# Windowed attention scores on one Trainium2 core: a block-diagonal 128x128 product becomes two 64x64 products, one for each head

## What is computed

```python
# attention: q, k, v are (4, 8, 576, 64) float32, batch x heads x positions x width
scores = scale * np.matmul(q, k.transpose(0, 1, 3, 2))
rel = pos[:, None] - pos[None, :]
mask = (rel >= 0) & (rel < 128)                  # a query sees itself and 127 keys before it
scores = np.where(mask, scores + bias[None], -1000000000.0)
attn = softmax(scores)                           # written out in the original
x = np.matmul(attn, v)                           # then rows of 512: 2304 tokens
# experts: each token goes to one of 8 experts with room for 288 each, by the sorted logits x @ w_gate
out[mask] = np.maximum(x[mask] @ w1[e], 0.0) @ w2[e]
# dense layer
h = x @ w_in
return (h * (1.0 / (1.0 + np.exp(-h)))) @ w_out
```

## Time and profile before

| | |
|---|---|
| median of three runs | 871.89 us |
| the profiled execution: its time, its span | 870.89 us, 868.9 us |
| TensorE matmul busy, share of the span | 828.4 us, 95% |
| VectorE busy | 502.3 us, 58% |
| ScalarE busy | 330.4 us, 38% |
| GpSimd busy | 300.4 us, 35% |
| score products, L435 | 60.3 us in 288 records, 339 ns each |
| transposes of queries, L580 | 24.5 us in 32 operations, 767 ns each |
| transposes of keys, L569 | 12.3 us in 16 operations, 770 ns each |

### The profile page before, as it was taken

How to read it: one execution, slowest core, us unless ns; L and a number is a source line. 1 busy time by engine, 2 the same in 40 slices (tenths; PEclk the granted TensorE clock), 3 DMA queues, 4 the chain that set the end, 5 groups by cost and what they waited for, 6 DMA issues and landing times.

```text
span 868.9 us, 17075 instructions
## 1 busy us (share of the span) xinstructions
PE 828.4 (95%) x6445; PEld 774.7 (89%) x6445; DVE 502.3 (58%) x1596; ACT 330.4 (38%) x767; POOL 300.4 (35%) x304
## 2 busy tenths in 40 slices
PE   5999999945999999999999999999999999999997
PEld 5999999834998998899899888998998899899996
DVE  7778788665756565566556343656566565542111
ACT  4655655413333432433343224333432433343221
POOL 1433333401424333623432334324423522443223
PEclk9999999865999999999999999999999999999999
DMA  9888888104204301240431030403210340421000
GB/s 150 171 173 171 164 185 185 55 15 147 76 2 125 97 26 46 81 122 1 126 91 32 1 118 8 134 2 125 85 38 22 104 122 2 125 84 39 1 1 36
DMA packets 154625, 71.38 MB, mean 82 GB/s; under 512 B 98992, under 2 KB 140976, under 8 KB 154544
## 3 DMA queue, kind: packets, MB, share of 16 engines
q1 hardware_dynamic: 149200, 60.56, 27.9%
q0 software_dynamic: 2976, 9.44, 3.5%
q10 hardware_dynamic: 2368, 0.30, 0.3%
HBM read 60.83 MB, written 9.44 MB: 81 GB/s over the span
## 4 chain that ended last, share of the span: by engine, by line
PE 71%; DVE 4%; DMA 1%; POOL 1%; issue 1%; ACT 0%; SPq 0%; POOLq 0%; DVEq 0%; ACTq 0%
PE hp L1124 12%; PE hp L1125 11%; PE hp L1126 11%; PE acc L1209 8%; PE acc L1211 8%; PE acc L1210 8%; PE acc L1124 4%; PE acc L1126 3%; PE acc L1125 3%; PE rt L1076 2%; DVE wa_l L1519 1%; DMA wa_raw<-in_moe_w_dram 1%; DVE test L1367 1%; PE rt L1091 0%; DVE test L1363 0%
## 5 line engine op out<-in xcount | busy, mean ns | idle before, releaser
L1052 POOL TENSOR_TENSOR h_l<-h_raw,h_h 128x256 fp32r<-128x256 f32 (+1 forms) x128 | 115.5, 902 | 264.4 <-ACT h_h L1324 264.2
L1588 DVE TENSOR_TENSOR h_raw<-hp,gate 128x256 f32<-128x256 f32 (+1 forms) x128 | 58.6, 457 | 181.7 <-ACT gate L1316 180.1
L1124 PE MATMUL hp<-xy_h,res_h 128*128 128x256 f32 (+1 forms) x512 | 154.0, 301 | 0.0
L1125 PE MATMUL hp<-xy_l,res_h 128*128 128x256 f32 (+1 forms) x512 | 151.4, 296 | 0.0
L1126 PE MATMUL hp<-xy_h,res_l 128*128 128x256 f32 (+1 forms) x512 | 151.2, 295 | 0.0
L1040 POOL TENSOR_TENSOR wb_l<-wb_raw,wb_h 128x512 fp32r<-128x512 f32 x64 | 85.3, 1334 | 132.7 <-ACT wb_h L1260 132.7
L1316 ACT ACTIVATE gate<-hp 128x256 f32<-128x256 f32 (+1 forms) x128 | 52.6, 411 | 196.3 <-PE hp L1126 181.5
L1209 PE MATMUL acc<-res_h,h_h 128*128 128x512 f32 x288 | 116.7, 405 | 0.0
L1211 PE MATMUL acc<-res_h,h_l 128*128 128x512 f32 x288 | 113.5, 394 | 0.0
L1210 PE MATMUL acc<-res_l,h_h 128*128 128x512 f32 x288 | 113.5, 394 | 0.0
L1124 PEld LDWEIGHTS hp<-xy_h,res_h 128*128 128x128 f32 x512 | 96.5, 188 | 3.6
(11 more groups left out here) (214 smaller groups left out, 1695.2 us busy)
## 6 DMA issues: line engine op xcount, KB each, us to landing
wa_raw<-in_moe_w_dram SPq DMA_DIRECT2D x64, 256.0 KB, 3.2
wb_raw<-in_moe_w_dram SPq DMA_DIRECT2D x64, 256.0 KB, 3.0
k_rows<-in_k_dram SPq DMA_DIRECT2D x64, 72.0 KB, 3.8
q_rows<-in_q_dram SPq DMA_DIRECT2D x60, 72.0 KB, 2.6
v_rows<-in_v_dram SPq DMA_DIRECT2D x32, 128.0 KB, 2.5
stage<-in_moe_w_in_dram SPq DMA_DIRECT2D x8, 512.0 KB, 4.6
x_rows<-x_rows_sb SPq DMA_DIRECT2D x16, 256.0 KB, 4.1
stage<-in_moe_w_out_dram SPq DMA_DIRECT2D x8, 512.0 KB, 4.4
```

The lines of the kernel that those rows point to most:

```text
L1052: pool.tensor_tensor(h_l[:, cols], h_raw[:, cols], h_h[:, cols].bitcast(FP32), ALU.subtract).then_inc(g_low, 1)
L1124: nc.tensor.matmul(out_, weights_h, cols_h, start=start, stop=False)
L1125: nc.tensor.matmul(out_, weights_h, cols_l, start=False, stop=False)
L1588: nc.vector.tensor_tensor(h_raw[:, h_cols(s, f)], hp[(A_NO[s, f] - 1) % 2][:, 0:width], gate[:, 0:width], ALU.mult).then_inc(g_done, 1)
```

## The change

Each unit's product with a block-diagonal weight tile is replaced by two products, one for each head, whose weights are 64x64. `tile_position=(0, 0)` puts the first head's into one quarter of the array, `(64, 64)` the second head's into the opposite quarter. Their results go to the same places of PSUM as before. Since the weights need no zeros, `qT` is as compact as `kT`, its buffers are not set to zero at the start, and the queries of both heads are turned by one operation of 128 partitions. The count in `q_turned` goes up once for a pair.

```diff
-        qT = [sb(f"qT{i}", [P, UNITS, P]) for i in range(2)]
+        qT = [sb(f"qT{i}", [P, S]) for i in range(2)]
...
-                    sp.wait_ge(q_turned, 2 * (g - RING_IN + 1))
+                    sp.wait_ge(q_turned, g - RING_IN + 1)
...
-            pool.memset(qT[1][:], 0.0).then_inc(pads_ready, 1)
...
-                        pe.wait_ge(q_turned, 2 * (g + 1))
+                        pe.wait_ge(q_turned, g + 1)
...
-                    last = nc.tensor.matmul(s_ps[s % 2][:, c:c + kw], qT[g % 2][:, u, :], kT[g % 2][:, k0:k0 + kw],
-                                            start=True, stop=True)
+                    for h in range(2):
+
+                        at = slice(U * h, U * (h + 1))
+                        last = nc.tensor.matmul(s_ps[s % 2][at, c:c + kw], qT[g % 2][at, U * u:U * (u + 1)],
+                                                kT[g % 2][at, k0:k0 + kw], start=True, stop=True,
+                                                tile_position=(U * h, U * h))
...
-            def turn_q(g, h):
+            def turn_q(g):
...
-                at = slice(U * h, U * (h + 1))
-                nc.vector.transpose(qT[g % 2][at, :, at],
-                                    q_rows[g % RING_IN][at].rearrange("p n d -> p (n d)").rearrange("p (u m) -> p u m", m=U)
-                                    ).then_inc(q_turned, 1)
+                nc.vector.transpose(qT[g % 2][:], q_rows[g % RING_IN][:].rearrange("p n d -> p (n d)")).then_inc(q_turned, 1)
...
-            nc.vector.memset(qT[0][0:U, :, U:P], 0.0)
-            nc.vector.memset(qT[0][U:P, :, 0:U], 0.0)
...
             turn_k(0)
-            turn_q(0, 0)
-            turn_q(0, 1)
+            turn_q(0)
             dve.wait_ge(bias_ready, PAIRS)
             bias_and_max(0)
             turn_k(1)
             bias_and_max(1)
-            turn_q(1, 0)
+            turn_q(1)
...
                 if kind == 3 and g + 2 < NG:
-                    turn_q(g + 2, 0)
-                if kind == 0 and g + 1 < NG:
-                    turn_q(g + 1, 1)
+                    turn_q(g + 2)
```

More of the change, by code:

```diff
@@ L479, in _ @@
             pe.wait_ge(ident_ready, 1)
-            pe.wait_ge(pads_ready, 4)
+            pe.wait_ge(pads_ready, 3)
             scores(0)
@@ L575, in turn_q @@
                     dve.wait_ge(s_done, 4 * (g - 1) + 1)
-                if (g, h) == (1, 0):
-                    dve.wait_ge(pads_ready, 4)
-                at = slice(U * h, U * (h + 1))
-                nc.vector.transpose(qT[g % 2][at, :, at],
-                                    q_rows[g % RING_IN][at].rearrange("p n d -> p (n d)").rearrange("p (u m) -> p u m", m=U)
-                                    ).then_inc(q_turned, 1)
+                nc.vector.transpose(qT[g % 2][:], q_rows[g % RING_IN][:].rearrange("p n d -> p (n d)")).then_inc(q_turned, 1)
             def add_logits(g):
```

## The result

The changed kernel takes 878.82 us (median of five runs, 877.80 to 879.48) against 871.72 us before (five runs beside them, 866.08 to 872.65). The ratio is 1.0094, with a 95% interval of 1.0062 to 1.0127. The forecast was 890.9 us, +19.0; measured are +7.1. The measured time lies inside the stated range (869 to 928) and near the lower end of the likeliest case's own (876 to 904), but the change is only 37% of the forecast one. The runs of the kernel before are less alike than those of the changed kernel; the fifth experiment shows why. The profiled execution after has a span of 877.7 us, 8.8 above that of before.

The account below looks back on a forecast made before the run. TensorE was taken to bound attention. Passes and change of shape 24.6, less 1.8, 0.8 and 3.0, gave +19.0 us; on the profiled 870.9 that is 889.9, with 1.0 for the median 890.9 us, range 869 to 928.

Parts of the forecast that it names:

- the likeliest case: Whole kernel: quarters overlap as five pass times a slot, with a middling shape-change price; chance 0.42, range 876 to 904.
- What bounds attention: Attention, 13 to 150 us: TensorE is full and others wait for it, so a slot's gain or loss counts 64 times.
- The passes: Score products of a slot: eight passes of 0.162 us take five pass times, one more than before, +10.4 us.
- A1 and A2 come before B1: Score products of a unit: the first head's two passes precede the second head's first pass in program order.
- the chain: Score passes of a slot: a head's second pass runs beside the other head's first; five times 0.162, +0.16 us.
- Full pairing: Score passes: both heads' first passes run together, a slot keeps four; 864.1 us with free shape change; rival, chance 0.15.
- The change of shape: Twice a slot, array between 128x128 and 64x64: costs 0, 0.11 or 0.44 us a slot, unknown which; middle taken.
- Narrower weights: 16 slots holding unit 0: loads of 64 columns take half, freeing two passes of 64 keys; -1.8 us.
- The start: Kernel start: one transpose of the queries instead of two, so TensorE starts 0.77 us earlier; -0.8 us.
- The clock: All of attention: smaller products drop the granted clock to 0.5, 137 us up to twice as long, towards 1010; rival, 0.03.
- The stall near 150 us: Around 150 us, where the ranking holds VectorE: TensorE's waits and its clock fall partly come back; -3.0 us, bounds 0 and -5.2.

Follow-up runs that it names:

- the fifth experiment: Changed kernel, two slots' scores together: 875.11 us; ranking's last two operations later, kernel before 866.37 us, changed kernel 877.38 us; changed kernel with both edits 871.50 us.
- the tiny products: Kernel before plus one 16-column product per slot, by weight tile: 64x64 895.69 us, 128x128 887.29 us, 64 rows by 128 columns 901.54 us, 128 by 64 893.84 us.

## Why the prediction was wrong

- **What bounds attention** was right. VectorE lost 16 us of work in the stretch and waited 16 us longer. What a slot gained or lost went through to the end.
- **The passes are the step that failed.** The prediction said that, since A1 and A2 come before B1, "the chain of a slot becomes" five passes, +0.16 us a slot, +10.4 us in all, and that the order of the program allows no more. A slot has four pairs and no fifth pass: the trace shows it, and one head alone has the same pitch. In the slots with two units it does not even matter whether the heads alternate. The term is 0. Full pairing was named as a rival and given 0.15, most of that with a free change of shape; what came, full pairing with a dearer one, had 0.02. What I took as evidence, that a head's two passes come from one instruction, did not hold B1 back: two passes start together, and since four passes of one head alone take a slot's whole time, the two are of two heads. The page of the Trainium skill named there, TensorE: Matmul & The Clock Gate, Part 3, has products in different tiles run at once, some 4 ns apart. The trace has two starts inside 0.03 us and agrees that they run at once; it is too coarse for the 4 ns.
- **The change of shape** was sized well. Without the chain, the middle between the free and the dearest price was 24.6 - 10.4 = 14.2 us, 0.22 us a slot. Measured: 0.13 to 0.30 in the four slots of a pair, 0.21 in the mean and 0.24 with the narrower weights set aside; 0.24 reckoned from the tiny products. It was called unknown, and it is what makes the change a loss. That a middle hit it is in part luck, since neither way of working it out fits: in the slot shown the end ahead of the scores cost 0.09 us, where the forecast had 0 or 0.16, and the end behind them 0.21, where it had 0.11 or 0.27. Why it is this much stays open.
- **Narrower weights**, -1.8 us: the pitch rose by 0.85, where four slots at 0.24 would give 0.96; the 0.11 between them is what 16 slots at 0.11 us gives, 1.8 us. The slot with unit 0 did grow least, 0.13. Consistent, not tested by itself.
- **The start**: 0.79 us earlier, and nothing of it left. The slot whose passes started at 13.00 before (in 0.65 us) had them at 12.42 (in 1.48), at what the lengths tell to be the lower clock level: the third slot's scores start at 15.01 us instead of 14.48.
- **The clock**: the forecast set its rival at 0.03, since the clock had fallen only after TensorE had waited. The changed kernel bore that out, but the reason is too weak: with one head's product left out it fell without a wait.
- **The stall near 150 us**, -3.0 forecast between 0 and -5.2: the wait is 1.0 instead of 1.8 us and the fall of the clock is gone. The pitch that holds the stall shows what both were worth: 15.43 us before against the usual 10.11, and 12.01 after against 10.98, so 5.3 and 1.0, which is -4.3.

The steps together, with the runs' numbers: 15 pitches at +0.85 are +12.8; the start +0.5 (15.01 less 14.48), the stall -4.3: +9.0, for a span that grew by 8.8. With the passes at 0 the forecast's own terms would have given 14.2 - 1.8 - 0.8 - 3.0 = +8.6 us, 880.5.

## What to carry to other kernels

Splitting a block-diagonal product over quarters of the array saves the zeros, and the quarters do run at once, surely so when the program has them by turns. But the full array did both heads in one product already, so nothing is won by it, and each trip to another tile shape and back cost 0.13 to 0.30 us here, which no other engine can hide when TensorE is the bound. So change the shape seldom, with much work between. When two kernels differ by less than 1%, look first for a stall that one of them has by chance of its timing: here 4 of 11 us were hidden by one.

## What the runs showed of the hardware that was not expected

- **The granted clock can fall though TensorE never waits.** With one 64x64 tile in the score passes it was 0.50 for the 95 us from 30 to 125 us, with TensorE busy all the time, and four runs spread from 882 to 995 us. With two 64x64 tiles at once, or one of 128x64, it was 1.00 from 13 to 150 us. What about the single quarter makes the difference, two kernels can't tell.
- **Passes of one tile need not wait for those of another that stand ahead in the program.** Eight passes took 0.81 us with the heads grouped and 0.80 with the heads by turns. With six passes of one head ahead it no longer held in full: twelve passes took 1.18 us instead of 0.81.
- **Tiles that share all their rows run at once too**: two 128x64 tiles, 8 passes in 0.80 us.
- **No weights were loaded ahead across a change of tile shape** in the slot shown: the load stood still for 0.17 us ahead of the scores and 0.28 us behind them.
